# Small f32 products of a chunked recurrence on four 64x64 tiles of TensorE, with loads, `grow`, `scale` and `norm` in other places

## The reference

```python
k_n = k / (np.linalg.norm(k, axis=-1, keepdims=True) + 1e-06)
state = 0                                     # [B, H, 48, 48]
for t in range(S):
    y[:, :, t] = q_t @ state
    v_old = k_t @ state
    state = state + b_t * outer(k_t, v_t - v_old)
x = y as [B, S, H * D]
x = moe(x)        # two FFTs, norm, 384 -> 1536 -> 384
out = moe2(x)     # angles, token mixing 768 x 768, 384 -> 384
```

## Time and profile before

| what | value |
|---|---|
| median of 3 runs | 892.65 us (891.03 to 893.04) |
| profiled execution | 890.82 us, of which 889.0 us span |
| mean granted TensorE clock | 0.974 |
| TensorE busy | 825.5 us (93%) |
| VectorE, ScalarE, GpSimd busy | 518.8, 343.1, 161.4 us |
| attention | 0 to about 301 us |

### The profile page before, as it was taken

One profiled execution on the slowest core, in us unless ns is written; L12 is line 12 of the kernel. 1 busy time (PEld: TensorE's weight loads), 2 busy tenths in 40 slices (PEclk: granted clock), 3 DMA queues, 4 the chain that ended last, 5 costly groups with the idle time before them and its releaser, 6 DMA issues.

```text
span 889.0 us, 24900 instructions
## 1 busy us (share of the span) xinstructions
PE 825.5 (93%) x11040; PEld 589.7 (66%) x11040; DVE 518.8 (58%) x1212; ACT 343.1 (39%) x659; POOL 161.4 (18%) x183
## 2 busy tenths in 40 slices
PE   5479897999989798999999999999999999999998
PEld 5479797989989555665566556665656666666664
DVE  5677768686756377362347244625554776867522
ACT  4356565556564225131314030503233453434311
POOL 5132313132210010120012001001221433323200
PEclk8699999899999899999999999999999999999999
DMA  8223423332211204101000101000000000000001
GB/s 196 54 51 69 134 49 71 70 74 58 58 39 35 78 28 138 49 1 54 1 27 27 54 1 37 18 1 1 1 1 1 1 28 10 27 18 27 28 27 54
DMA packets 60984, 37.69 MB, mean 42 GB/s; under 512 B 45641, under 2 KB 57292, under 8 KB 60876
## 3 DMA queue, kind: packets, MB, share of 16 engines
q1 hardware_dynamic: 52612, 30.95, 12.8%
q10 hardware_dynamic: 8264, 5.15, 2.2%
HBM read 26.65 MB, written 4.72 MB: 35 GB/s over the span
## 4 chain that ended last, share of the span: by engine, by line
PE 80%; DVE 7%; ACT 6%; issue 4%; DMA 1%; ACTq 1%; SPq 0%; DVEq 0%
PE bank L291 13%; PE bank L1036 5%; PE bank L1084 5%; PE bank L1082 5%; PE bank L1083 5%; PE bank L1038 5%; PE bank L1037 5%; PE bank L330 4%; PE bank L1020 3%; PE bank L1022 3%; PE bank L1021 3%; PE bank L970 2%; DVE hT_lo L1454 2%; PE bank L358 2%; PE bank L976 2%
## 5 line engine op out<-in xcount | busy, mean ns | idle before, releaser
L1202 ACT ACTIVATE hT_hi<-bank 128x384 f16<-128x384 f32 x96 | 46.8, 489 | 160.9 <-PE bank L1022 160.8
L1036 PE MATMUL bank<-wA,hT_hi 128*128 128x384 f16 x288 | 94.0, 326 | 2.8 <-DVE hT_lo L1454 2.8
L1454 DVE SCALAR_TENSOR_TENSOR hT_lo<-bank,hT_hi 128x384 f16<-128x384 f32 x96 | 53.2, 555 | 73.7 <-ACT hT_hi L1202 73.4
L1020 PE MATMUL bank<-unT,wA 128*128 128x384 f16 x288 | 93.9, 326 | 0.3 <-DVE hT_lo L1454 0.3
L1022 PE MATMUL bank<-unT,wA 128*128 128x384 f16 x288 | 93.9, 326 | 0.0
L1021 PE MATMUL bank<-unT,wA 128*128 128x384 f16 x288 | 93.9, 326 | 0.0
L1038 PE MATMUL bank<-wA,hT_lo 128*128 128x384 f16 x288 | 93.9, 326 | 0.0
L1037 PE MATMUL bank<-wA,hT_hi 128*128 128x384 f16 x288 | 93.9, 326 | 0.0
L291 PE MATMUL bank<-Yv,ET 64*64 64x48 f32 x2304 | 76.2, 220 | 6.0 <-issue 3.9
L291 PEld LDWEIGHTS bank<-Yv,ET 64*64 64x64 f32 x2304 | 71.8, 136 | 9.3 <-issue 5.2
L278 POOL TENSOR_TENSOR AP<-AP,mP 128x256 f32<-128x256 f32 x48 | 36.2, 773 | 178.4 <-ACT AP L438 178.2
(11 more groups left out here) (202 smaller groups left out, 1781.7 us busy)
## 6 DMA issues: line engine op xcount, KB each, us to landing
Kb<-k_dram SPq DMA_DIRECT2D x12, 384.0 KB, 5.5
Vv<-v_dram SPq DMA_DIRECT2D x12, 384.0 KB, 3.7
z_first<-w_dram SPq DMA_DIRECT2D x8, 576.0 KB, 4.0
z_first<-wt_dram SPq DMA_DIRECT2D x8, 576.0 KB, 3.6
out_dram<-hT_hi SPq DMA_DIRECT2D x24, 192.0 KB, 1.8
KQ<-q_dram SPq DMA_DIRECT2D x44, 96.0 KB, 4.1
X<-Yo ACTq DMA_DIRECT2D x12, 192.0 KB
X<-Yo ACTq DMA_DIRECT2D x10, 189.0 KB
```

Source lines behind the costliest of these rows:

```text
L1020: pe.matmul(out, w1[0][:, k, cols], unT[0][:, k, :], start=(k == 0), stop=False)
L1036: pe.matmul(out, hT[0][:, f, cols], w2[0][:, f, :], start=(f == 0), stop=False)
L1454: dve.scalar_tensor_tensor(hT[1][:, f, :], bank[3 + m % 3][:, 0:TG * P], 0.0, hT[0][:, f, :], ALU.max, ALU.subtract).then_inc(s_hl, 1)
```

## The change

Heads are paired anew: keys `Kb` lie as [m, r], so that column block m holds group m of the first set in feature half r = 0, and group m of the second set in r = 1. The rows' half `r` of a tile is then also the set, that is, the PSUM bank into which a product goes. (For the state the bank goes by `h`.) In `gram`, `predicted`, the query products and the growth the four tiles of `TILES` follow one another inside a single loop over m, and the semaphores between straight and crossed products are gone; one completion is signalled for both banks instead of one for each. `gram(c+2)` now runs over the banks (0, 2) and (1, 3).

On TensorE `corner(c, 0)` goes ahead of `predicted(c)`; `outputs` falls into `queried` (query products), `direct` (P times Y) for each set and `grow`, which goes between the two `direct`s, and which the last chunk leaves out. On VectorE the first `mask_e` goes ahead of `make_x`, and `norm` and, from chunk 0 on, `scale` go behind `scaled_u`. On SyncE the queries' loads wait for the first hop and the keys' for the third; the queries' DMAs have the same bytes in longer contiguous pieces, the keys of a chunk come in two DMAs. GpSimd's squares come in two halves for each chunk.

```diff
-        KQ = sb("KQ", [P, RT, 2, HG, 2, C])
+        KQ = sb("KQ", [P, RT, 2, 2, HG, C])
-        Kb = sb("Kb", [P, RK, NG, C])
+        Kb = sb("Kb", [P, RK, HG, 2, C])
...
-            for kind, n, parts in (("E", c, (0, 1)), ("GP", c + 2, (0, 1)), ("GP", c + 2, (2, 3)), ("T", c + 3, (0, 1)),
+            for kind, n, parts in (("E", c, (0, 1)), ("GP", c + 2, (0, 2)), ("GP", c + 2, (1, 3)), ("T", c + 3, (0, 1)),
...
-        STRAIGHT, CROSSED = ((0, 0), (1, 1)), ((1, 0), (0, 1))
+        TILES = ((0, 0), (1, 1), (0, 1), (1, 0))
...
-                        sp.wait_ge(s_S, 2 * (n - RK + 1))
-                    sp.dma_start(Kb[:, n % RK, :, 0:D], A["k"][:, n]).then_inc(s_kd[n % RK], 16)
+                        sp.wait_ge(s_S, n - RK + 1)
+                    for r in range(2):
+                        sp.dma_start(keys(n, r), A["k"][:, n, grp(r)]).then_inc(s_kd[n % RK], 16)
...
-                        q = A["q"][h, :, n].rearrange("d (m r) t -> r d m t", r=2)
                         for r in range(2):
-                            sp.dma_start(KQ[feat[r], n % RT, 1, :, h, :], q[r]).then_inc(s_qd[n % RT], 16)
+                            sp.dma_start(KQ[feat[r], n % RT, 1, h], A["q"][h, :, n, grp(r)]).then_inc(s_qd[n % RT], 16)
...
                 load_v(c + 2 if c + 2 > 1 else -1)
+                if c >= 0:
+                    sp.wait_ge(s_Y, 8 * c + 4)
                 load_q(c + 3 if c + 3 > 2 else -1)
+                if c >= 0:
+                    sp.wait_ge(s_Y, 8 * c + 8)
                 load_k(c + 5 if c + 5 > 3 else -1)
...
-                    k = Kb[:, n % RK, :, 0:D]
-                    pool.tensor_tensor(kk[:, n % 2], k, k, ALU.mult).then_inc(s_kk, 1)
+                    for r in range(2):
+                        pool.tensor_tensor(kk[:, n % 2, grp(r)], keys(n, r), keys(n, r), ALU.mult).then_inc(s_kk, 1)
...
-                for tiles in (STRAIGHT, CROSSED):
-                    for u in parts:
-                        if tiles is STRAIGHT:
-                            out = take("GP", n, u)
-                        else:
-                            out = ring("GP", n, u)
-                            pe.wait_ge(s_gs, 4 * n + u + 1)
-                        for m in (2 * u, 2 * u + 1):
-                            for h, r in tiles:
-                                j = 2 * m + r - 4 * u
-                                mm = pe.matmul(out[half[h], j * P:(j + 1) * P], KQ[feat[r], n % RT, 0, m, h, :],
-                                               KQ[feat[r], n % RT, :, m, h, :], start=True, stop=True, skip_group_check=True)
-                        mm.then_inc(s_gs if tiles is STRAIGHT else s_gp, 1)
+                out = [take("GP", n, u) for u in parts]
+                for j in range(HG // 2):
+                    m = parts[0] * HG // 2 + j
+                    for h, r in TILES:
+                        mm = pe.matmul(out[r][half[h], j * P:(j + 1) * P], KQ[feat[r], n % RT, 0, h, m],
+                                       KQ[feat[r], n % RT, :, h, m], start=True, stop=True, skip_group_check=True)
+                mm.then_inc(s_gp, 1)
...
+                pe.wait_ge(s_se, 2 * c)
+                for m in range(HG):
+                    for h, r in TILES:
+                        mm = pe.matmul(chain(r)[half[h], m * D:(m + 1) * D], KQ[feat[r], c % RT, 0, h, m],
+                                       Sv[feat[r], c % 2, h * HG + m], start=m == 0, stop=True, skip_group_check=True)
+                mm.then_inc(s_X, 1)
...
+            def queried(c):
...
+                out = [take("O", c, a)[:, 0:HG * D].rearrange("p (g d) -> p g d", g=HG) for a in range(2)]
+                if c:
+                    for m in range(HG):
+                        for h, r in TILES:
+                            mm = pe.matmul(out[r][half[h], m], KQ[feat[r], c % RT, 1, h, m], Sv[feat[r], c % 2, h * HG + m],
+                                           start=m == 0, stop=False, skip_group_check=True)
+                    mm.then_inc(s_oq, 1)
+                return out
+
+            def direct(c, a, out):
...
+                pe.wait_ge(s_pt, 4 * c + 4)
+                pe.wait_ge((s_ya, s_yd)[a], 4 * c + 4)
+                if c:
+                    pe.wait_ge(s_oq, c)
+                for j in range(HG):
+                    g = a * HG + j
+                    mm = pair(out[a][:, j], PT[:, c % RA, g], Yv[:, c % 2, g], c == 0 and j == 0, True)
+                mm.then_inc(s_O, 1)
+
+            def grow(c):
+                if not 0 <= c < LAST:
+                    return
...
+                for m in range(HG):
+                    for h, r in TILES:
+                        mm = pe.matmul(state(h)[feat[r], m * D:(m + 1) * D], key(c, h, r, m), Yv[half[h], c % 2, r * HG + m],
+                                       start=c == 0 and m == 0, stop=True, skip_group_check=True)
+                mm.then_inc(s_S, 1)
...
             for c in range(C0, NC):
+                corner(c, 0)
                 predicted(c)
-                corner(c, 0)
                 corner(c, 1)
                 solve(c)
-                gram(c + 2, (0, 1))
+                gram(c + 2, (0, 2))
                 hop(c, 1)
-                gram(c + 2, (2, 3))
+                gram(c + 2, (1, 3))
                 hop(c, 2)
                 turn(c + 3)
                 hop(c, 3)
-                outputs(c)
+                out = queried(c)
+                direct(c, 0, out)
+                grow(c)
+                direct(c, 1, out)
...
+                act.wait_ge(s_S, c + 1)
                 for a in range(2):
-                    act.wait_ge(s_S, 2 * c + a + 1)
                     copy(flat(Sv[:, (c + 1) % 2], a), state(a)).then_inc(s_se, 1)
...
+                mask_e(c, 0)
                 make_x(c)
-                mask_e(c, 0)
                 mask_e(c, 1)
                 blocks_in(c + 1)
                 eliminate(c + 1, (1, 2, 3, 4, 5, 6, 7))
                 if c < 0 and c % 2 == 0:
                     scale((c + 2) // 2)
+                eliminate(c + 1, (8, 9, 10, 11, 12, 13, 14))
+                scaled_u(c + 1)
                 if c % 2:
                     norm((c + 3) // 2)
                 elif c >= 0:
                     scale((c + 2) // 2)
-                eliminate(c + 1, (8, 9, 10, 11, 12, 13, 14))
-                scaled_u(c + 1)
                 blocks_out(c + 1)
```

More of the change, by code:

```diff
@@ L178, in flat, with keys, key @@
             return t[:, grp(a)].rearrange("p g d -> p (g d)")
-        STRAIGHT, CROSSED = ((0, 0), (1, 1)), ((1, 0), (0, 1))
-        def heads(a, tiles):
-            return [(h, 2 * m + r, m, r) for m in range(4 * a, 4 * a + 4) for h, r in tiles]
+        TILES = ((0, 0), (1, 1), (0, 1), (1, 0))
+        def keys(n, r):
+            return Kb[:, n % RK, :, r, 0:D]
+        def key(n, h, r, m):
+            return Kb[half[h], n % RK, m, r, 0:D]
         def moves_of(c):
@@ L273, in mask_p @@
                     pool.wait_ge(s_cst, 16 * 5)
-                for u in range(4):
-                    pool.wait_ge(s_ab, 4 * n + u + 1)
+                for i, u in enumerate((0, 2, 1, 3)):
+                    pool.wait_ge(s_ab, 4 * n + i + 1)
                     p = PT[:, n % RA, 4 * u:4 * u + 4]
@@ L302, in turn @@
                     return
[L303 removed]
+                pe.wait_ge(s_kd[n % RK], 32 * (n // RK + 1))
                 if n == 0:
@@ L390, in outputs @@
                     pe.wait_ge(s_zs, 2)
-                for tiles in (STRAIGHT, CROSSED):
-                    for a in range(2):
-                        if tiles is STRAIGHT:
-                            pe.wait_ge((s_ya, s_yd)[a], 4 * c + 4)
-                        else:
-                            pe.wait_ge(s_ss, 2 * c + a + 1)
-                        for i, (h, g, m, r) in enumerate(heads(a, tiles)):
-                            j = 2 * (m - 4 * a) + h
-                            mm = pe.matmul(state(a)[feat[r], j * D:(j + 1) * D], Kb[half[h], c % RK, g, 0:D],
-                                           Yv[half[h], c % 2, g], start=c == 0 and tiles is STRAIGHT and i < 2, stop=True,
-                                           skip_group_check=True)
-                        mm.then_inc(s_ss if tiles is STRAIGHT else s_S, 1)
@@ L403, in outputs @@
-                pe.wait_ge(s_pt, 4 * c + 4)
-                out = [take("O", c, a)[:, 0:HG * D].rearrange("p (g d) -> p g d", g=HG) for a in range(2)]
-                if c:
-                    for a in range(2):
-                        for i, (h, g, m, r) in enumerate(heads(a, CROSSED)):
-                            mm = pe.matmul(out[a][half[h], g - HG * a], KQ[feat[r], c % RT, 1, m, h, :],
-                                           Sv[feat[r], c % 2, 2 * m + h], start=i < 2, stop=False, skip_group_check=True)
-                        mm.then_inc(s_oc, 1)
@@ L411, in outputs @@
[L411 to L420 removed]
+                for a in range(2):
+                    pe.wait_ge((s_ya, s_yd)[a], 4 * c + 4)
```

59 lines of the change are left out of this document (18 added, 41 removed).

## The result

| | before | after |
|---|---|---|
| median, beside each other | 892.85 us (891.03 to 894.81) | 907.5 us (906.51 to 908.95, 4 runs) |
| profiled execution, span | 890.8, 889.0 us | 906.9, 905.0 us |
| mean granted TensorE clock | 0.974 | 0.962 |
| TensorE busy | 825.5 us | 808.8 us |
| `To`, first and last start | 33.4, 282.1 us | 33.8, 294.8 us |

The ratio is 1.0165 [1.0138, 1.0192]. The time lies in the forecast range (883 to 911) and on the forecast side, but the loss is 14.65 us where 5.4 were forecast (898.0 against 892.65).

A forecast was written before the change was run, and what follows sets the result against it. Two nearly equal attention loops, TensorE's and that of TT, bound the kernel. Nine chunks -4.6, half clock +14.3, c=0 -3.5, c=10 +1 and last chunk -1 gave +6.2 us on 890.8, 897.0; it said 898, range 883 to 911.

The forecast's parts named there:

- the mechanism: At each chunk's start TensorE waits 4.4 us for TT ahead of corner, with half clock behind the wait.
- ledger: The forecast's step-by-step sum through one chunk at full clock; both masks done 3.85 us after corner starts.
- The four tiles: TensorE's narrow products start about 14 ns apart for predicted and queries, 27 gram, 13 grow; 3.6 us saved per chunk.
- The step that failed: Attention chunk: TensorE's path of 21.9 us lies beside VectorE's, so the full-clock period is 22.2 us for all.
- the better spreading: Waits inside TensorE's hops may go with the spreading; that gain is already in the period, with no separate size.
- the full-clock period: Nine middle chunks take 22.2 us each against 22.7 on average, 4.6 us won in all.
- Half clock: Behind the wait ahead of corner, 1.3 us lost per chunk (bounds 0 and 1.8), +14.3 us in eleven chunks.
- The last chunk: At the attention's end, dropping grow and half its queries' time but gaining predicted in the loop: -1 us.
- The dense part: The rest behind the attention is untouched by the change and keeps its time: 0 us.
- Rival 2: Attention: TensorE's clock holds or falls mostly inside the wait; 883 to 884 us, partial losses 880 to 892; chance 0.33.
- Rival 3: TensorE's narrow products keep 20 or 26 ns for want of faster instructions; 908 to 918 us; chance 0.13.
- Rival 4: GpSimd's squares and values meet VectorE's first part, 1.5 us every second chunk; +7 on the forecast, 905 us; chance 0.08.

The follow-up runs named there:

- a1: Changed kernel with predicted ahead of both corners on TensorE and make_x ahead of both masks on VectorE again: 891.73 us, 0.998.
- f1: Changed kernel with only TensorE's order put back, predicted ahead of both corners: 890.41 us, 0.9957.
- a3: Changed kernel with 16 unused identity products ahead of corner in each chunk from c=1 on: 899.68 us, 1.0075.
- b3: A follow-up run; the text ties this label to no described change or time.
- d1: Changed kernel with GpSimd's masks held until VectorE has finished setting up blocks: 905.38 us, 1.0135.
- f2: Changed kernel with only VectorE's order put back, make_x ahead of both masks: 911.26 us, 1.0196.
- e6: Changed kernel with unused small products ahead of chunk 6, 256 on four tiles, then 128 on two: 933.41 us, one execution.
- e5: Changed kernel with unused small products behind the attention, 256 on four tiles, then 256 on two: 941.03 us, one execution.
- c1: Changed kernel with predicted and make_x first, grow first and norm between the elimination's halves again: 882.24 us, 0.9856.
- a4: Kernel before with only the new pairing, layouts, four alternating tiles and longer load pieces: 894.08 us, 1.0015.

## Why the prediction was right in direction and too small

**Right: the mechanism.** The loss is a wait for `TT` ahead of `corner` in every chunk, 3.7 to 4.8 us long (forecast 4.4), with half clock behind it. It comes from the order at the start of a chunk (a1: all 15 us), from TensorE's half of it (f1), and the added dependence has the forecast size, both masks at 3.87 us (ledger 3.85). The four tiles run at the forecast pace; `scale` takes 2.9 us behind `Us` in c=0, 2 and 4 (147.88 to 150.82) and 3.7 and 3.8 in c=6 and 8, where GpSimd works beside it (forecast 3.9, bound 3.0); in c=1, 5 and 7 ScalarE's `Sv` waits for `norm`'s root (it is complete 1.7 to 1.8 us after `grow` instead of 0.94), as was said.

The changed kernel's rows of c=4 by which these are read, ScalarE's and VectorE's in one timeline:

```profile
133.62 0.69 DVE L663 TENSOR_TENSOR ET<-bank,mE 128x512 f32<-128x512 f32 x1 [4.45 <-PE bank L298]
...
136.19 0.68 DVE L663 TENSOR_TENSOR ET<-bank,mE 128x512 f32<-128x512 f32 x1
...
141.72 1.07 PE L298 MATMUL bank<-Yv,ET 64*64 64x48 f32 x30 [1.39 <-issue]
...
147.44 0.60 DVE L647 TENSOR_TENSOR Us<-bank,cT 128x256 f32<-128x256 f32 x1
147.88 0.16 DVE L579 TENSOR_SCALAR nr<-nr 128x32 f32<-128x32 f32 x1
...
150.57 0.25 DVE L592 SCALAR_TENSOR_TENSOR cT<-cx,rows,cT 128x32 f32<-128x32 f32 x1
...
152.08 0.87 ACT L436 ACTIVATE Sv<-bank 128x384 f32<-128x384 f32 x2 [2.51 <-PE bank L413]
...
153.78 0.71 DVE L655 STREAM_TRANSPOSE To<-Ux 128x512 f32<-128x512 f32 x1 [2.95 <-ACT Ux L436]
```

**The step that failed** is the sum of TensorE's path and its place below VectorE's: "14.0 ... 17.1 ... 21.9. This path lies beside VectorE's, so that TensorE's gain is not felt beyond it. The period at full clock is 22.2 us for all". In a3's chunks at full clock `grow` ends 17.6 to 18.2 us after `corner` starts, not 17.1, and with `Sv`, `Ux`, `To` and `TT` behind it (4.9 us to the next `corner`, 5.05 in c=2) the period is 22.8. In four of these five chunks `Sv` starts at once behind `grow`, and `To` at once behind `Ux`. VectorE's loop, 3.87 + 12.1 + 2.9 + 3.0 = 21.9, is the shorter one, except in c=2, where `scale` ran beside GpSimd's squares: it was sized about rightly and put first wrongly. Of the 0.8 us that TensorE's path is longer, 0.2 is a slip in the sum: by the earlier trace rows the third hop ends 14.7 us after `corner` (143.12 + 2.07 - 130.47), not 14.5. What fits the rest are TensorE's stalls for instructions, 0.5 to 0.9 us ahead of `grow`'s end in each of those chunks, which the ledger left out; no run takes them away, so this part is argued and not shown. The forecast took the better spreading as a gain "in it already"; there was none: unexplained stalls outside `corner` add up to 7.4 us against 5.8 before. A faster row of products reaches the end of what has been fetched sooner.

**By terms.** Nine chunks: the full-clock period 22.8 instead of 22.2, so +0.1 x 9 and not -4.6: 5.5 us of the miss. Half clock: 1.5 instead of 1.3 per chunk, +1.8. Together they are the 14.3 measured against 7.1. (The upper bound was 1.8. By the same five chunks of both kernels it is 1.4, and more of the miss falls to the period.) c=0 gained 1.7 more than forecast: its clock stayed full. The last chunk (+0.5, forecast -1) was not taken apart. The dense part's +2.7 was not foreseen: it begins with half clock, and that lasts 13.7 us instead of 6.8. The same 13.7 us stand in b3, d1, f2 and e6, and 6.8 in the others but e5, whose added products stand there; why is open. The loss goes with it: the dense part takes 591.0 to 591.7 us in those with 13.7, and 588.3 to 590.0 in those with 6.8. The forecast had it that the change touches nothing there.

**The rivals.** Rival 2 (the clock holds) is refuted by the windows and by 54.6 us at half clock. Rival 3 said that the narrow products would get no faster for want of instructions. In its own terms it is wrong, they start 12 to 15 ns apart; but what it said of the long run, that instructions don't come fast enough, is seen in the pauses. The Trainium skill ("TensorE: Matmul & The Clock Gate", "Wait — 56ns, not 53.3ns?") has products never start less than about 25 ns apart. The traces here disagree with it inside a row (14.6 ns); a row of 128 with its pause averages 29. Rival 4 (GpSimd meets VectorE) exists, 0.9 us in the elimination, and costs nothing that can be measured here (d1).

## What to carry to other kernels

When two loops share a chunk, sum each of them from its own rows, stalls included, before saying which one hides the other: less than 1 us decided here, and an order that adds 1.0 us to the dependence and then a stall pays 1.4 to 1.5 us more for the clock. Ask also what stands in the half-clock stretch: work that is waited for pays, work done during the wait doesn't. Products shortened below the rate at which instructions arrive give their time back as pauses; look whether an engine's stalls "for issue" grow when its busy time falls. And try each moved piece alone: `scale` moved by two lines gave 1.3%, from which the whole change at its best can't be told apart.

## What the hardware showed unexpectedly

- TensorE's instructions arrive in pieces of 16 KB (128 weight loads and 128 products), whose starts are at least 3.25 us apart in every trace here. A row of short products stops for 0.3 to 2.5 us at a piece's end; stalls outside `corner` that no semaphore explains add up to 5.8 us before, 7.4 in the changed kernel, and in the versions whose `corner` waits less 16.9 (a1), 16.6 (c1) and 21.0 us (a4).
- Such pauses alone are followed by half clock: in e6 after one of 0.93 and in one of 1.65 us, in a row that waits for no other engine.
- Four 64x64 tiles of f32 products each keep their own pace: 28 ns between starts for `gram`'s 128 columns, 14.6 for 48 columns, 12 with 48-column weights.
- VectorE's short steps on SBUF wait for GpSimd: `scale` took 5.6 to 6.8 us beside two of GpSimd's squares in c=0 to 6 of the kernel before and 2.9 alone.
